# Two 64-row matmuls on the two halves of the TensorE array, in a kernel of causal convolution and rational feed-forward

## The chip, the cores and the metric

One NeuronCore of a Trainium2 chip runs the kernel. The metric is the device time of one execution in microseconds (us), the median of three runs. Durations of single instructions come from one execution that was recorded by the hardware profiler.

## What is computed

For every token and each of 8 heads, softmax weights over 7 taps mix the token's own 24 values of the head with those of the six tokens before it (zeros ahead of a sequence). The result, 16,384 rows of 192 values, goes through a feed-forward stage whose activation is a ratio of polynomials.

```python
w = exp(weight_gen - max); w = w / (sum(w) + 1e-9)          # (4, 4096, 8, 7)
out[b, s, h, :] = sum_k w[b, s, h, k] * x_pad[b, s + k, h, :]  # x (4, 4096, 192), 6 zeros ahead
h = out.reshape(16384, 192) @ w_in                            # w_in (192, 2048)
P = a[0] + a[1] * h + a[2] * h**2 + a[3] * h**3
Q = 1.0 + abs(b[0]) * abs(h) + abs(b[1]) * h**2
g = P / (Q + 1e-06)
return g @ w_out                                              # w_out (2048, 192)
```

## The kernel before, in words

**Tiles.** Each of the 128 partitions holds 128 tokens; a tile takes 4 tokens of each, 512 in all (`COLS`), so there are 32 tiles. The 2048 hidden units are 16 chunks of 128, in six groups of 3, 2, 3, 3, 2 and 3 chunks (`GROUP_CHUNKS`). A chunk's h is 128 units x 512 tokens, one PSUM bank; six banks (`hps`) hold two groups in turn, two more (`ops`) the output of the tile.

**The first product.** The 192 inputs are split in 128 and 64. To keep precision, weights and inputs are each split into a part that the fast float32r format holds exactly (hi) and a rest (lo). The 64-row remainder of the inputs stands in one tensor, `xt_hl`: hi in partitions 0 to 63, lo in 64 to 127, and the 64 last rows of the weights (`wi_hi[:, 1]`, `wi_lo[:, 1]`) are there twice, once in each half. Each chunk so takes five matmuls of 128 rows (`first_product`, L669 to L681): hi·hi, lo·hi and hi·lo of the first 128 inputs, then `wi_hi[:, 1]` and, as the fifth, `wi_lo[:, 1]` against `xt_hl`. The fifth so adds lo·hi from the upper half and lo·lo, the smallest term, from the lower. A matmul instruction loads its own weights first (LDWEIGHTS, "PEld" in the rows).

**The order of work.** It is written out by hand for each engine, with semaphores between them. In `tile` (L696) TensorE does for each group q: the transposes of the next tile's inputs, where they are due (`transpose1` at q = 1, `transpose0` at q = 4), the first product of group q, and the second product of the group four places earlier (`back`, L725, `second_product`, L683: per chunk four matmuls with 192 columns, L690). Before group q it waits until VectorE has used the h of group q-2 (`h_used`, L705). Before the second product at q = 4 it waits until ScalarE has copied the previous tile's output out of `ops` (`out_ready`, L729). That copy (`evacuate`, L441) stands in ScalarE's order at q = 3, after the Ln of L452, and waits for TensorE's second product at q = 3.

**The other engines.** ScalarE (ACT) reads a group's h three times where the square goes through it (q = 0, 2, 3, 5: L471, L474, L479) and twice otherwise (L476, L479), and inverts the denominator two groups back (`invert`, L449: L452 and L455). It waits for the h at the first of these (`h_ready`) and for the gate of the group four back (`gate_ready`, L466). VectorE (DVE) finishes the gate of the group three back (L605), does two steps of the numerator (L621, L624), and, for q = 1 and 4, a product of the denominator (L629). `lo_part1` (L570) writes the lo half of `xt_hl` for the next tile, at q = 1, ahead of that group's gate. GpSimd (POOL) does the convolution (L323, L327), the other step of the denominator (L353) and issues the accumulating DMAs (L346).

Of the kernel before, what the change touches and what calls it, by code (L numbers as in the profile page):

```python
# [25 lines left out]
F32R = mybir.dt.float32r  # L26
# [4 lines left out]
P = 128  # L31
GROUP_CHUNKS = (3, 2, 3, 3, 2, 3)
GROUPS = len(GROUP_CHUNKS)
GROUP_START = tuple(sum(GROUP_CHUNKS[:q]) for q in range(GROUPS))
# [14 lines left out]
def conv_rational_ffn(nc, x, weight_gen, w_in, w_out, a, b, out):  # L49
# [7 lines left out]
    COLS = TOK * P  # L57
    HALO = TAPS - 1
    D1 = D - P
# [19 lines left out]
    with ctx:  # L79
        def sb(name, shape, dt=F32):  # L80
            return ctx.enter_context(nc.sbuf_tensor(name, shape, dt))

        def sem(name):
            return ctx.enter_context(nc.semaphore(name))


        wi_hi = sb("wi_hi", [P, 2, FF], F32R)
        wi_lo = sb("wi_lo", [P, 2, FF], F32R)
# [14 lines left out]
        xt_hi = [sb(f"xt_hi{n}", [P, COLS], F32R) for n in range(2)]  # L103
        xt_lo = [sb(f"xt_lo{n}", [P, COLS], F32R) for n in range(2)]
        xt_hl = [sb(f"xt_hl{n}", [P, COLS], F32R) for n in range(2)]
        num = sb("num", [P, RING, GW])

        wi_stage = num[:, :, :].rearrange("p r w -> p (r w)")[:, 0:2 * FF].rearrange("p (n f) -> p n f", n=2)
# [7 lines left out]
        hps = ctx.enter_context(nc.psum_tensor("hps", [P, 6, COLS], F32))  # L116
# [6 lines left out]
        def place(odd, q, lag=0):  # L123

            return (GROUPS * odd + q - lag) % (2 * GROUPS)
# [50 lines left out]
        xt_ps1 = sem("xt_ps1")  # L176
        xt_hi_ready = sem("xt_hi_ready")
        xt_lo_ready = sem("xt_lo_ready")
        h_ready = sem("h_ready")
        abs_ready = sem("abs_ready")  # L180
        lin_ready = sem("lin_ready")
# [324 lines left out]
        def _(dve):  # L506
# [5 lines left out]
            def pre_softmax_start(s, parity):  # L512

                dve.wait_ge(taps_loaded[parity], after_dmas(s, parity))
                dve.tensor_reduce(out=tap_max[parity][:, :], in_=per_head(taps_raw[parity]), op=ALU.max,
                                  axis=AX.X).then_inc(pre_max, 1)
                dve.wait_ge(pre_max, s + 1)
                dve.tensor_tensor(per_head(taps[parity]), per_head(taps_raw[parity]), over_taps(tap_max[parity]),
                                  ALU.subtract).then_inc(pre_sub, 1)
# [50 lines left out]
            def lo_part1(s, parity, bank):  # L570

                dve.wait_ge(xt_hi_ready, 2 * s + 1)
                dve.tensor_tensor(xt_hl[parity][D1:P, :], bank[0:D1, :],
                                  xt_hl[parity][0:D1, :].bitcast(F32), ALU.subtract).then_inc(xt_lo_ready, 1)

            pre_softmax_start(0, 0)
            pre_softmax_start(1, 1)
# [12 lines left out]
            dve.wait_ge(conv_steps, CONV_STEPS)  # L590
            pre_softmax_start(2, 0)
            lo_part1(0, 0, hps[:, BANK1, :])
            lo_part0(0, 0)
            wi_lo_half(1)
# [13 lines left out]
            def tile(t, odd, first=False, xt_ahead=True, taps_ahead=True):  # L608
                for q in range(GROUPS):
# [4 lines left out]
                    if first and q == FIRST_XT1 - 1:  # L614
                        lo_part1(t + 1, 1 - odd, ops[:, 0, :])
                    if xt_ahead and q == XT1 and not first:
                        lo_part1(t + 1, 1 - odd, hps[:, BANK1, :])
# [35 lines left out]
        @block.tensor  # L653
        def _(pe):
            def transpose0(parity):

                for j in range(TOK):
                    last = pe.transpose(hps[:, BANK0, j * P:(j + 1) * P],
                                        conv[parity][:, j * D:j * D + P], ident[:, :])
                last.then_inc(xt_ps0, 1)  # L660

            def transpose1(parity, bank):

                for j in range(TOK):
                    last = pe.transpose(bank[0:D1, j * P:(j + 1) * P],  # L665
                                        conv[parity][:, j * D + P:(j + 1) * D], ident[:, :])
                last.then_inc(xt_ps1, 1)

            def first_product(q, parity, very_first=False):  # L669

                for n in range(GROUP_CHUNKS[q]):
                    units = slice((GROUP_START[q] + n) * P, (GROUP_START[q] + n + 1) * P)
                    to = hps[:, 3 * (q % 2) + n, :]
                    terms = ((wi_hi[:, 0, units], xt_hi[parity]), (wi_lo[:, 0, units], xt_hi[parity]),
                             (wi_hi[:, 0, units], xt_lo[parity]), (wi_hi[:, 1, units], xt_hl[parity]),
                             (wi_lo[:, 1, units], xt_hl[parity]))
                    for m, (w, xt) in enumerate(terms):
                        if very_first and n == 0 and m == 2:
                            pe.wait_ge(xt_lo_ready, 2)
                        last = pe.matmul(to, w, xt[:, :], start=(m == 0), stop=(m == len(terms) - 1))  # L680
                last.then_inc(h_ready, 1)  # L681

            def second_product(g):  # L683


                q = g % GROUPS
                for n in range(GROUP_CHUNKS[q]):
                    c = GROUP_START[q] + n
                    for j in range(TOK):
                        last = pe.matmul(ops[:, j // 2, (j % 2) * D:(j % 2 + 1) * D],  # L690
                                         gate[:, g % GATE_RING, n * COLS + j * P:n * COLS + (j + 1) * P],
                                         wo[:, c, :], start=(c == 0 and j % 2 == 0), stop=(c == CHUNKS - 1),
                                         skip_group_check=True)
                last.then_inc(gate_used, 1)

            def tile(t, odd, first=False, xt_ahead=True):  # L696
                if first:
                    pe.wait_ge(wi_lo_ready, 1)
                    pe.wait_ge(xt_hi_ready, 2)
                else:  # L700
                    pe.wait_ge(xt_lo_ready, 2 * t + 2)
                for q in range(GROUPS):
                    i = GROUPS * t + q
                    if not first or q >= 2:
                        pe.wait_ge(h_used, i - 1)  # L705
                    if first and GROUP_START[q] == CHUNKS // 2:
                        pe.wait_ge(wi_lo_ready, 2)
                    if xt_ahead and q == (FIRST_XT1 if first else XT1):
                        pe.wait_ge(conv_steps, CONV_STEPS * (t + 2))
                        if first:  # L710
                            pe.wait_ge(conv_by_dve, 2 * CONV_STEPS)
                        pe.sem_inc(pe_passed, 1)
                        transpose1(1 - odd, ops[:, 0, :] if first else hps[:, BANK1, :])
                    if xt_ahead and not first and q == XT1 + 2:
                        pe.wait_ge(xt_lo_ready, 2 * t + 3)
                    if xt_ahead and q == XT0:
                        transpose0(1 - odd)
                    first_product(q, odd, first and q == 0)
                    if first and q == LAG:
                        pe.wait_ge(xt_lo_ready, 3)  # L720
                        pe.wait_ge(wo_loaded, 16)
                    if not first or q >= LAG:
                        back(t, odd, q, first)

            def back(t, odd, q, first=False):  # L725

                pe.wait_ge(gate_ready, GROUPS * t + q - LAG + 1)
                if q == LAG and not first:
                    pe.wait_ge(out_ready, t)  # L729
                second_product(place(odd, q, LAG))  # L730

            pe.wait_ge(ident_ready, 2)
            pe.wait_ge(conv_steps, CONV_STEPS)
            pe.wait_ge(conv_by_dve, CONV_STEPS)
            transpose1(0, hps[:, BANK1, :])
            transpose0(0)
            tile(0, 0, first=True)
            with pe.Fori(1, TILES - 1, 2) as t:
                tile(t, 1)
                tile(t + 1, 0)  # L740
            tile(TILES - 1, (TILES - 1) % 2, xt_ahead=False)
            for q in range(LAG):
                back(TILES, TILES % 2, q)
# [21 lines left out]
```

## Time and profile before

| | |
|---|---|
| median of 3 runs | 1422.62 us (1420.06 to 1422.7) |
| the profiled execution | 1420.86 us |
| its span, first to last instruction | 1419.1 us |
| PE (TensorE matmul) | 1307.0 us busy, 92% |
| PEld (weight loads) | 1178.2 us, 83% |
| ACT | 1270.7 us, 90% |
| DVE | 1214.8 us, 86% |
| POOL | 1036.6 us, 73% |
| mean granted TensorE clock | 0.992 |

The busy times are those of the whole span. Matmuls are pipelined: the recorded duration of one is longer than the distance to the next, so a rate is read from the starts. The page's chain (the work that ended last, followed back) gives 62% of the span to PE, 25% to ACT, 7% to "issue" (time in which the engine waited for nothing that the profile shows) and 4% to DVE.

### The profile page before, as it was taken

What the parts mean: (1) busy time and instruction counts of PE and PEld (TensorE: products, weight loads), DVE (VectorE), ACT (ScalarE), POOL (GpSimd) and SP (SyncE); (2) the same over time, 40 slices, a digit from 0 to 9 for tenths busy, and PEclk for the clock granted to TensorE, in tenths of its full rate; (3) what the DMA queues carried; (4) which work ended last, traced back from release to release, by engine and by line L of the source; (5) the groups of instructions that cost most, each with busy time, mean ns of one, the idle gap of its engine ahead of it and who ended that gap; (6) DMA issues with size and microseconds to landing.
All of it is one profiled execution on the core that took longest, in us unless ns stands there. A gap on an engine that the chain in (4) does not pass through costs nothing.

```text
span 1419.1 us, 19150 instructions
## 1 busy us (share of the span) xinstructions
PE 1307.0 (92%) x6912; PEld 1178.2 (83%) x6912; DVE 1214.8 (86%) x872; ACT 1270.7 (90%) x1030; POOL 1036.6 (73%) x672
## 2 busy tenths in 40 slices
PE   0279999999999999999999999999999999999997
PEld 0268898888898888889888888988888888888897
DVE  2988898899889889989888998988988898898775
ACT  1278999999999999999999999999999999999995
POOL 1878787787878778878777887877788787787210
PEclk9889999999999999999999999999999999999999
DMA  2534444534544544454454354445345445533432
GB/s 89 144 90 110 103 117 114 128 85 107 131 94 114 125 117 88 115 120 105 109 131 107 87 126 108 117 109 131 87 102 131 97 117 120 119 83 81 100 68 67
DMA packets 35486, 152.21 MB, mean 107 GB/s; under 512 B 3992, under 2 KB 10260, under 8 KB 35472
## 3 DMA queue, kind: packets, MB, share of 16 engines
q0 software_dynamic: 18432, 100.67, 34.9%
q1 hardware_dynamic: 16752, 51.36, 10.5%
q8 instruction: 7, 0.11, 0.0%
q10 hardware_dynamic: 288, 0.00, 0.0%
q14 instruction: 7, 0.06, 0.0%
HBM read 38.78 MB, written 12.58 MB: 36 GB/s over the span
## 4 chain that ended last, share of the span: by engine, by line
PE 62%; ACT 25%; issue 7%; DVE 4%; DMA 2%; SPq 0%; ACTq 0%; DVEq 0%
PE ops L690 33%; PE hps L680 28%; ACT num L479 7%; ACT beta L474 6%; ACT den L452 6%; ACT den L471 4%; DMA xwin<-in_x 2%; ACT out_sb L446 2%; PE hps L665 1%; DVE gate L543 1%; DVE conv L554 1%; ACT den L455 1%; DVE gate L605 0%; DVE wi_lo L561 0%; DVE num L621 0%
## 5 line engine op out<-in xcount | busy, mean ns | idle before, releaser
L690 PE MATMUL ops<-wo,gate 128*128 128x192 f32 x4096 | 702.2, 327 | 41.7 <-ACT out_sb L446 35.8
L690 PEld LDWEIGHTS ops<-wo,gate 128*128 128x128 f32 x4096 | 676.0, 191 | 69.8 <-issue 48.5
L621 DVE TENSOR_TENSOR num<-num,hps 128x1536 f32<-128x1536 f32 (+1 forms) x192 | 301.6, 1571 | 153.4 <-ACT num L479 153.4
L327 POOL TENSOR_TENSOR conv<-conv,prod 128x768 f32<-128x768 f32 (+2 forms) x192 | 395.2, 2058 | 15.0
L605 DVE SCALAR_TENSOR_TENSOR gate<-num,coef,den 128x1536 f32<-128x1536 f32 (+1 forms) x192 | 375.0, 1953 | 2.6 <-issue 1.6
L323 POOL TENSOR_TENSOR prod<-xwin,taps 128x768 f32<-128x768 f32 (+2 forms) x192 | 336.7, 1754 | 3.4
L624 DVE SCALAR_TENSOR_TENSOR num<-num,coef,hps 128x1536 f32<-128x1536 f32 (+1 forms) x192 | 314.2, 1637 | 6.8
L346 POOL DMA_DIRECT2D den<-beta x128 | 112.7, 881 | 265.8 <-ACT beta L474 260.3
L479 ACT ACTIVATE num<-hps,coef 128x1536 f32<-128x1536 f32 (+1 forms) x192 | 287.8, 1499 | 0.0
L452 ACT ACTIVATE den<-den,one_eps 128x1536 f32<-128x1536 f32 (+1 forms) x192 | 277.8, 1447 | 0.0
L471 ACT ACTIVATE den<-hps,absb 128x1536 f32<-128x1536 f32 x128 | 196.6, 1536 | 77.1 <-PE hps L680 70.5
L455 ACT ACTIVATE den<-den 128x1536 f32<-128x1536 f32 (+1 forms) x192 | 259.0, 1349 | 4.2
L680 PE MATMUL hps<-xt_hi,wi_hi 128*128 128x512 f32 x512 | 226.0, 441 | 2.8 <-ACT xt_hi L415 2.8
L680 PE MATMUL hps<-xt_lo,wi_hi 128*128 128x512 f32 x512 | 203.1, 397 | 0.0
L680 PE MATMUL hps<-xt_hi,wi_lo 128*128 128x512 f32 x512 | 203.0, 397 | 0.0
L680 PE MATMUL hps<-xt_hl,wi_lo 128*128 128x512 f32 x512 | 203.0, 396 | 0.0
L680 PE MATMUL hps<-xt_hl,wi_hi 128*128 128x512 f32 x512 | 202.7, 396 | 0.0
L474 ACT ACTIVATE beta<-hps,root 128x1536 f32<-128x1536 f32 x128 | 196.8, 1538 | 0.0
L353 POOL TENSOR_SCALAR beta<-den,absb 128x1024 f32<-128x1024 f32 x64 | 136.6, 2134 | 41.3 <-ACT den L476 24.8
L680 PEld LDWEIGHTS hps<-xt_lo,wi_hi 128*128 128x128 f32 x512 | 96.9, 189 | 23.3 <-DVE xt_lo L567 0.5
L680 PEld LDWEIGHTS hps<-xt_hl,wi_hi 128*128 128x128 f32 x512 | 97.1, 190 | 22.7
L680 PEld LDWEIGHTS hps<-xt_hl,wi_lo 128*128 128x128 f32 x512 | 97.0, 189 | 22.8
(52 smaller groups left out, 766.5 us busy)
## 6 DMA issues: line engine op xcount, KB each, us to landing
den<-beta POOLq DMA_DIRECT2D x128, 768.0 KB, 5.6
xwin<-in_x SPq DMA_DIRECT2D x30, 960.0 KB
out<-out_sb SPq DMA_DIRECT2D x32, 384.0 KB, 3.8
taps_raw<-in_weight_gen SPq DMA_DIRECT2D x32, 112.0 KB, 3.9
wo<-in_moe_w_out SPq DMA_DIRECT2D x1, 1536.0 KB, 13.6
num<-in_moe_w_in SPq DMA_DIRECT2D x2, 512.0 KB, 6.6
num<-in_moe_w_in SPq DMA_DIRECT2D x4, 256.0 KB, 7.9
xwin<-in_x SPq DMA_DIRECT2D x1, 768.0 KB
```

Source lines behind the costliest of these rows:

```text
L323: pool.tensor_tensor(to[:, first_head:, :], shifted(xwin[parity], k)[:, first_head:, :], tap(taps[parity], k)[:, first_head:, :], ALU.mult ...
L327: pool.tensor_tensor(conv[parity][:, cols], conv[parity][:, cols], prod[k % 2][:, cols], ALU.add).then_inc(conv_steps, 1)
L452: act.activation(slot(den, g), slot(den, g), ACT.Ln, bias=one_eps[:, 0:1]).then_inc(ln_ready, 1)
L455: act.activation(slot(den, g), slot(den, g), ACT.Exp, scale=-1.0).then_inc(inv_q_ready, 1)
L471: act.activation(slot(den, g), h_of(q), ACT.Abs, scale=absb[:, 0:1]).then_inc(abs_ready, 1)
L474: act.activation(slot(beta, g), h_of(q), ACT.Square, scale=root[:, 2:3]).then_inc(square_ready, 1)
L479: act.activation(slot(num, g), h_of(q), ACT.Identity, scale=coef[:, 3:4], bias=coef[:, 2:3]).then_inc(lin_ready, 1)
L605: dve.scalar_tensor_tensor(slot(gate, g), slot(num, g), coef[:, 0:1], slot(den, g), ALU.add, ALU.mult).then_inc(gate_ready, 1)
L621: dve.tensor_tensor(slot(num, g), slot(num, g), h_of(q), ALU.mult).then_inc(num2_ready, 1)
L624: dve.scalar_tensor_tensor(slot(num, g), slot(num, g), coef[:, 1:2], h_of(q), ALU.add, ALU.mult).then_inc(h_used, 1)
L680: last = pe.matmul(to, w, xt[:, :], start=(m == 0), stop=(m == len(terms) - 1))
L690: last = pe.matmul(ops[:, j // 2, (j % 2) * D:(j % 2 + 1) * D], gate[:, g % GATE_RING, n * COLS + j * P:n * COLS + (j + 1) * P], wo[:, c, ...
```

## The change

The fifth matmul of the first two chunks of every group takes 64 rows in place of 128. Chunk 0's uses partitions 0 to 63 (`wi_lo` times the hi half of `xt_hl`); chunk 1's uses partitions 64 to 127, against a new tensor `xt_h2`, whose lower half holds a copy of the same hi half. The two follow each other directly and write two banks. The third chunk of a group keeps its fifth matmul of 128 rows. For the copies VectorE gets one more instruction a tile, behind the one in `lo_part1`. For chunks 0 and 1 the term lo·lo is no longer added.

```diff
@@ VectorE, lo_part1
                 dve.tensor_tensor(xt_hl[parity][D1:P, :], bank[0:D1, :],
                                   xt_hl[parity][0:D1, :].bitcast(F32), ALU.subtract).then_inc(xt_lo_ready, 1)
+                dve.tensor_copy(xt_h2[parity][D1:P, :], xt_hl[parity][0:D1, :]).then_inc(xt_h2_ready, 1)
@@ TensorE, first_product
-                for n in range(GROUP_CHUNKS[q]):
-                    units = slice((GROUP_START[q] + n) * P, (GROUP_START[q] + n + 1) * P)
-                    to = hps[:, 3 * (q % 2) + n, :]
-                    terms = ((wi_hi[:, 0, units], xt_hi[parity]), (wi_lo[:, 0, units], xt_hi[parity]),
-                             (wi_hi[:, 0, units], xt_lo[parity]), (wi_hi[:, 1, units], xt_hl[parity]),
-                             (wi_lo[:, 1, units], xt_hl[parity]))
-                    for m, (w, xt) in enumerate(terms):
-                        if very_first and n == 0 and m == 2:
-                            pe.wait_ge(xt_lo_ready, 2)
-                        last = pe.matmul(to, w, xt[:, :], start=(m == 0), stop=(m == len(terms) - 1))
+                def term(n, m, w, xt, stop=False):
+                    if very_first and n == 0 and m == 2:
+                        pe.wait_ge(xt_lo_ready, 2)
+                    return pe.matmul(hps[:, 3 * (q % 2) + n, :], w, xt, start=(m == 0), stop=stop)
+
+                def units(n):
+                    return slice((GROUP_START[q] + n) * P, (GROUP_START[q] + n + 1) * P)
+
+                def full_terms(n):
+                    term(n, 0, wi_hi[:, 0, units(n)], xt_hi[parity][:, :])
+                    term(n, 1, wi_lo[:, 0, units(n)], xt_hi[parity][:, :])
+                    term(n, 2, wi_hi[:, 0, units(n)], xt_lo[parity][:, :])
+                    term(n, 3, wi_hi[:, 1, units(n)], xt_hl[parity][:, :])
+
+                full_terms(0)
+                full_terms(1)
+                term(0, 4, wi_lo[0:D1, 1, units(0)], xt_hl[parity][0:D1, :], stop=True)
+                last = term(1, 4, wi_lo[D1:P, 1, units(1)], xt_h2[parity][D1:P, :], stop=True)
+                if GROUP_CHUNKS[q] == 3:
+                    full_terms(2)
+                    last = term(2, 4, wi_lo[:, 1, units(2)], xt_hl[parity][:, :], stop=True)
                 last.then_inc(h_ready, 1)
@@ TensorE, tile
                 if first:
                     pe.wait_ge(wi_lo_ready, 1)
                     pe.wait_ge(xt_hi_ready, 2)
+                    pe.wait_ge(xt_h2_ready, 1)
                 else:
                     pe.wait_ge(xt_lo_ready, 2 * t + 2)
+                    pe.wait_ge(xt_h2_ready, t + 1)
```

On TensorE, the first product of a group of three chunks, before (shapes are those of the outputs, 128 units x 512 tokens; `wi_hi` and `wi_lo` the weights, `xt_hi`, `xt_lo`, `xt_hl` the inputs of the tile, its parity number behind them):

```order
L680 MATMUL hps<-xt_hi1,wi_hi 128x512
L680 MATMUL hps<-xt_hi1,wi_lo 128x512
L680 MATMUL hps<-xt_lo1,wi_hi 128x512
L680 MATMUL hps<-xt_hl1,wi_hi 128x512
L680 MATMUL hps<-xt_hl1,wi_lo 128x512
L680 MATMUL hps<-xt_hi1,wi_hi 128x512
L680 MATMUL hps<-xt_hi1,wi_lo 128x512
L680 MATMUL hps<-xt_lo1,wi_hi 128x512
L680 MATMUL hps<-xt_hl1,wi_hi 128x512
L680 MATMUL hps<-xt_hl1,wi_lo 128x512
L680 MATMUL hps<-xt_hi1,wi_hi 128x512
```

and the same place now:

```order
L677 MATMUL hps<-xt_hi1,wi_hi 128x512
L677 MATMUL hps<-xt_hi1,wi_lo 128x512
L677 MATMUL hps<-xt_lo1,wi_hi 128x512
L677 MATMUL hps<-xt_hl1,wi_hi 128x512
L677 MATMUL hps<-xt_hi1,wi_hi 128x512
L677 MATMUL hps<-xt_hi1,wi_lo 128x512
L677 MATMUL hps<-xt_lo1,wi_hi 128x512
L677 MATMUL hps<-xt_hl1,wi_hi 128x512
L677 MATMUL hps<-xt_hl1,wi_lo 128x512
L677 MATMUL hps<-xt_h21,wi_lo 128x512
L677 MATMUL hps<-xt_hi1,wi_hi 128x512
```

The number of matmuls is the same; chunk 0's fifth moved behind chunk 1's fourth, next to chunk 1's fifth, and these two have 64 rows each.

On VectorE, tile 1 onward, between group q = 0's last step and group q = 1's first, before:

```order
L624 SCALAR_TENSOR_TENSOR num<-num,coef,hps 128x1536
L631 ISA
L632 TENSOR_REDUCE tap_max<-taps_raw 128x32
L572 ISA
L573 TENSOR_TENSOR xt_hl<-hps,xt_hl 64x512
L601 REGISTER_ALU
L604 REGISTER_ALU
L605 SCALAR_TENSOR_TENSOR gate<-num,coef,den 128x1024
```

and now:

```order
L627 SCALAR_TENSOR_TENSOR num<-num,coef,hps 128x1536
L634 ISA
L635 TENSOR_REDUCE tap_max<-taps_raw 128x32
L574 ISA
L575 TENSOR_TENSOR xt_hl<-hps,xt_hl 64x512
L577 COPY xt_h<-xt_hl 64x512
L604 REGISTER_ALU
L607 REGISTER_ALU
L608 SCALAR_TENSOR_TENSOR gate<-num,coef,den 128x1024
```

The copy (L577) is the one new instruction there, ahead of the gate of q = 1. Ahead of the first tile it stands between `lo_part1` and `lo_part0` in the same way.

## Rows read from the trace of the kernel before

**Rows 1.** Waits of the whole span: us in total, times, longest.
```profile
DVE num L621 <- ACT num L479: 153.4, 97, 4.0
ACT den L471 <- PE hps L680: 70.5, 64, 3.8
...
PE ops L690 <- ACT out_sb L446: 35.8, 31, 1.5
```
**Rows 2.** One tile: us; busy PE, PEld, DVE, ACT, POOL; granted clock; DMA.
```profile
677.63:719.32 41.69, 40.78 (x217) 36.52 (x217) 37.66 (x27) 39.50 (x33) 33.16 (x22) 1.00 0.47 112
```
**Rows 3.** Chain that ended last, in that tile: start us, us, what.
```profile
677.63 4.14 PE ops L690 x24
681.77 3.49 PE hps L680 x15
...
701.92 3.51 PE hps L680 x15
...
719.32 4.14 PE ops L690 x24
```
**Rows 4.** The same chain, the same step in the first and the last such tile.
```profile
135.77 4.14 PE ops L690 x24
...
1385.74 4.14 PE ops L690 x24
```
**Rows 5.** ACT's timeline in that tile; in brackets idle before, and releaser.
```profile
682.43 1.49 ACT L455 ACTIVATE den<-den 128x1536 f32<-128x1536 f32 x1
685.30 1.54 ACT L471 ACTIVATE den<-hps,absb 128x1536 f32<-128x1536 f32 x1 [1.38 <-PE hps L680]
...
703.27 1.49 ACT L455 ACTIVATE den<-den 128x1536 f32<-128x1536 f32 x1
705.45 1.54 ACT L471 ACTIVATE den<-hps,absb 128x1536 f32<-128x1536 f32 x1 [0.68 <-PE hps L680]
...
712.95 1.54 ACT L471 ACTIVATE den<-hps,absb 128x1536 f32<-128x1536 f32 x1
```
**Rows 6.** DVE's timeline in that tile; the first row is of the tile before.
```profile
675.79 1.75 DVE L621 TENSOR_TENSOR num<-num,hps 128x1536 f32<-128x1536 f32 x1 [1.43 <-ACT num L479]
...
697.19 1.75 DVE L621 TENSOR_TENSOR num<-num,hps 128x1536 f32<-128x1536 f32 x1 [1.80 <-ACT num L479]
...
701.12 0.69 DVE L573 TENSOR_TENSOR xt_hl<-hps,xt_hl 64x512 fp32r<-64x512 f32 x1
...
708.17 3.40 DVE L605 SCALAR_TENSOR_TENSOR gate<-num,coef,den 128x1536 f32<-128x1536 f32 x1
...
717.47 1.76 DVE L621 TENSOR_TENSOR num<-num,hps 128x1536 f32<-128x1536 f32 x1 [0.65 <-ACT num L479]
```
**Rows 7.** Groups by line and shape: count, busy us, mean ns, idle before.
```profile
L509 DVE MEMSET xwin<- 128x384 f32 x1 | 0.4, 378 | 0.0
```
**Rows 8.** PE and PEld in the middle of a first product, timeline.
```profile
702.22 0.39 PE L680 MATMUL hps<-xt_lo,wi_hi 128*128 128x512 f32 x1
702.22 0.19 PEld L680 LDWEIGHTS hps<-xt_hl,wi_hi 128*128 128x128 f32 x1
702.45 0.39 PE L680 MATMUL hps<-xt_hl,wi_hi 128*128 128x512 f32 x1
```
**Rows 9.** PE, then PEld, around the transposes with a 128*64 part of the array.
```profile
691.68 3.58 PE L690 MATMUL ops<-wo,gate 128*128 128x192 f32 x21
695.09 0.60 PE L665 MATMUL hps<-ident,conv 128*64 128x128 f32 x4
695.45 0.48 PE L680 MATMUL hps<-xt_hi,wi_hi 128*128 128x512 f32 x1
...
695.42 0.19 PEld L680 LDWEIGHTS hps<-xt_hi,wi_hi 128*128 128x128 f32 x1
695.53 0.19 PEld L680 LDWEIGHTS hps<-xt_hi,wi_lo 128*128 128x128 f32 x1
```
**Rows 10.** Chain that ended last, one step before the first tile.
```profile
49.29 0.69 DVE xt_hl L573
```

More of the change, by code:

```diff
@@ L105, in conv_rational_ffn @@
         xt_hl = [sb(f"xt_hl{n}", [P, COLS], F32R) for n in range(2)]
+        xt_h2 = [sb(f"xt_h2{n}", [P, COLS], F32R) for n in range(2)]
         num = sb("num", [P, RING, GW])
@@ L178, in conv_rational_ffn @@
         xt_lo_ready = sem("xt_lo_ready")
+        xt_h2_ready = sem("xt_h2_ready")
         h_ready = sem("h_ready")
```

## The prediction

> **What bounds the kernel now.** I began with the shares of the engines: PE 92%, ACT 90%, DVE 86%. So close together they name no bound, and the waits come next. [rows 1] show DVE idle 153.4 us for ACT, ACT idle 70.5 us for TensorE (64 times, two a tile) and TensorE idle only 35.8 us, 31 times, once a tile, for ACT's copy of the output. TensorE and ACT hold each other. In one tile [rows 2] TensorE's busy time is 40.78 of 41.69 us, ACT's 39.50; the granted clock is 1.00, the 2.4 GHz level.
>
> The chain of that tile [rows 3] says how. It starts at 677.63, when the output copy lets TensorE go on, and stays on TensorE to 701.92 + 3.51 = 705.43: second products and four first products, those of q = 5, 0, 1 and 2 (two of them stand in the rows, besides the last). Then it goes over to ACT, which starts on the h of q = 2 at 705.45 [rows 5], works through to the output copy, and TensorE starts again at 719.32. So 27.8 us of the 41.69 belong to TensorE, and the rest to ACT. The same step is at 135.77 in the first such tile and at 1385.74 in the last [rows 4]: 1249.97 us, 30 periods of 41.67. What a faster TensorE is worth is read from this period.
>
> Two other ways through the tile are nearly as long. **Path B:** ACT starts on q = 5 at 685.30, after 1.38 us of waiting for TensorE, then works without a gap to 703.27 + 1.49 = 704.76 and waits 0.68 us for q = 2 [rows 5]. Only one of the four first products lies ahead of that start. **Path C:** from the same start ACT feeds DVE, which begins at 697.19 [rows 6] on the numerator of q = 0 and is busy to the end of the gate at 708.17 + 3.40 = 711.57. ACT needs that gate for q = 3, which it starts at 712.95 [rows 5]: 1.38 us of slack.
>
> **The pair.** Call s what TensorE saves per group where two 64-row matmuls take the place of two of 128 rows. Matmuls of 512 columns start 0.23 us apart (702.22, 702.45) though each is recorded with 0.39 [rows 8]; a first product of three chunks takes 3.49 us for 15 [rows 3], 0.233 us each. If the two halves run side by side, one such step goes away: s = 0.23. No trace of this kernel shows two matmuls side by side, so the bounds are wide. The upper is 0.23, since the pair must take at least the one. What could eat into it is the weight loads: the pair still needs two. A load starts with the previous matmul (702.22 both) and the next matmul starts 0.23 later [rows 8]. The tightest distance of two loads in the rows is 0.11 us (695.42 to 695.53) [rows 9], so two fit into one step of 0.23 if the load for the lower half may start ahead of the matmul of the upper one. If it may not, the second matmul starts 0.11 late: s = 0.12. By the recorded length of a load, 0.19 [rows 8], s would be 0.04. The lower bound, below nothing, is in the rivals. I take 0.23: both loads go to rows that the running matmul's successor doesn't yet use, and nothing in the trace holds a load back but its place.
>
> The Trainium skill (TensorE: Matmul & The Clock Gate, "Measured speedup vs the span model") has tiles in different row groups run together at 4 ns more per further tile, which no row here shows; s would be 0.228.
>
> **What it is worth in the period.** Path A, the present chain, holds four pairs: 41.69 - 4s. Path B holds one: 41.69 - 0.68 - s = 41.01 - s. Path C holds one, and the new copy, of c us, stands in its DVE stretch, right behind the row at 701.12 [rows 6]: 41.69 - 1.38 - s + c = 40.31 - s + c. The pairs of q = 3 and 4 lie beside ACT's part of the chain; they only lengthen the wait for the output copy, 35.8 / 31 = 1.15 us a tile [rows 1], and are worth nothing.
>
> **The copy.** c is not in the trace. The nearest row is the 64x512 subtract just ahead of it, 0.69 us, which reads PSUM too [rows 6]; a write without any source takes 0.378 us for 384 columns [rows 7], 0.50 for 512 by proportion. I take 0.65, near the subtract, since both read and write the same shape. Beside a busy POOL it may be longer: the gate at 708.17 takes 3.40 us where another step of the same shape takes 1.76 [rows 6]; by that ratio c could reach 1.3. The copy is queued ahead of the gate of q = 1 and all of DVE's work up to 717.47, where DVE has 0.65 us of waiting to take it up; in the tile before, the same wait is 1.43 [rows 6], so every other tile has 0.78 more room on path C.
>
> With s = 0.23 and c = 0.65 the three paths give 40.77, 40.78 and 40.73. The period becomes **40.78**, 0.91 less by path B, and the three are tied. ACT would be busy 39.50 of it [rows 2], nearly the next bound. Thirty periods: 27.3 us.
>
> **Start and end.** Ahead of 135.77 the chain goes through three first products of tiles 0 and 1, and through one behind 1385.74: 4 x 0.23 = 0.9 less. Ahead of the first tile the chain is on DVE, and the copy stands in it, right behind the subtract at 49.29 [rows 10]: 0.65 more. Together 0.3 less. TensorE's added waits on the copy cost nothing: the copy is done right after 701.12, and the next tile's first product is due after 719.32 and the whole of q = 4 and 5. The four matmuls of chunk 1 that now come ahead of chunk 0's fifth cost nothing either: the group is handed over by one semaphore at its end, as before.
>
> **Sum.** 1420.86 - 27.3 - 0.3 = 1393.3 for the profiled execution. That stands 1.8 below the median of the runs, so I forecast **1395.0**. Own range of this case: 1389 (path B giving way a little) to 1404 (c = 1.3 lets path C bind at 41.38 in every other tile; 15 x 0.6 = 9 more).
>
> **Rivals.**
>
> *The loads come one behind the other.* s = 0.12 gives path A 41.21, path B 40.89: 0.48 a tile, 14.4 in 30, so 1408; s = 0.04 gives 0.16 a tile and 1418. For it speaks that a load never starts ahead of the previous matmul in [rows 8]; against it, that those all use the same rows of the array.
>
> *The halves don't run side by side at all,* the change then does not do what it says: s = 0, path A stays, and the copy at the start is added: 1423. Nothing in the trace speaks against it but the sense of the array; the matmuls have always been in order.
>
> *The array must run empty where the height of its parts changes,* ahead of the pair and behind it. The price is from [rows 8]: recorded 0.39, distance 0.23, so 0.16 us by which each matmul outlasts the start of the next. Twice 0.16 less the 0.23 of the pair makes s = -0.09; path A grows by 4 x 0.09 = 0.36 a tile, 30 times: 1422.6 + 10.8 + 0.65 = 1434. It decides from 0.115 us a change on. If in addition the halves don't overlap, s = -0.32 and it is 1462. Against it speaks a change of part that the trace has: the transposes with 128*64 start at 695.09, while the last of 21 second products is recorded to 691.68 + 3.58 = 695.26, and the next full matmul starts at 695.45, while the last transpose is recorded to 695.69 [rows 9]. Neither change let the array run empty. But that part is narrower, not lower, and 64 rows are not in the trace. The Trainium skill (TensorEngine Tiling (Array Packing), "Key Properties") says that changing the tiling mode, not merely the tile, drains the engine. By that rule the sum would be the 1434 of this rival; for the width of a part the trace disagrees, for the height nothing here shows it.
>
> **Chances.** Side by side with s near 0.23: 0.60. Loads in the way, 1404 to 1418: 0.14. No overlap: 0.10. Array run empty: 0.16. A measurement of this kernel tells about 0.2% from no change, 2.8 us: below 1419.8 it is faster, above 1425.5 slower. Faster is 0.60 + 0.14 = 0.74, same 0.10, slower 0.16. The range goes from 1389 to 1425 and leaves out the drained array, 0.16, and little at the low end.
>
> **What the profile would show.** If I am right: the second matmul of each pair starts within 0.02 us of the first, the three-chunk first product takes about 3.26 us in place of 3.49, the period of the output copy is 40.8, TensorE's wait for that copy grows by about 0.46 a tile, ACT's wait of 0.68 ahead of q = 2 shrinks to nearly nothing while that ahead of q = 5 stays, and DVE's of 0.65 at 717.47 is gone. The prediction is wrong if the pair's starts are 0.1 to 0.2 apart (loads) or 0.39 after the matmul before (array empty), if the step behind the pair is longer than 0.23, or if ACT is found waiting for a gate of DVE ahead of q = 3.

## The result, and the profile after

| | before | after |
|---|---|---|
| median | 1422.22 us (4 runs) | 1440.86 us (4 runs, 1440.74 to 1441.14) |
| ratio | | 1.0137, 95% interval 1.0121 to 1.0153 |
| the profiled execution, its span | 1420.86, 1419.1 | 1441.14, 1439.3 |
| PE, PEld busy | 1307.0, 1178.2 | 1331.7, 1128.6 |
| ACT, DVE busy | 1270.7, 1214.8 | 1271.0, 1231.3 |

The change costs 18.6 us. I had forecast 27 us less. The first look goes to the pair itself, in the timelines of PE and PEld after the change (start us, duration, engine, line, operands; the part of the array stands ahead of the shape):

```profile
710.90 0.40 PE L677 MATMUL hps<-xt_hl,wi_hi 128*128 128x512 f32 x1
711.23 0.50 PE L677 MATMUL hps<-xt_hl,wi_lo 64*128 64x512 f32 x1
711.24 0.49 PE L677 MATMUL hps<-xt_h,wi_lo 64*128 64x512 f32 x1
711.66 0.50 PE L677 MATMUL hps<-xt_hi,wi_hi 128*128 128x512 f32 x1
712.00 0.39 PE L677 MATMUL hps<-xt_hi,wi_lo 128*128 128x512 f32 x1
```
```profile
710.67 0.19 PEld L677 LDWEIGHTS hps<-xt_hl,wi_hi 128*128 128x128 f32 x1
711.23 0.18 PEld L677 LDWEIGHTS hps<-xt_hl,wi_lo 64*128 64x128 f32 x1 [0.37 <-issue]
711.23 0.18 PEld L677 LDWEIGHTS hps<-xt_h,wi_lo 64*128 64x128 f32 x1
711.66 0.19 PEld L677 LDWEIGHTS hps<-xt_hi,wi_hi 128*128 128x128 f32 x1 [0.24 <-issue]
711.77 0.19 PEld L677 LDWEIGHTS hps<-xt_hi,wi_lo 128*128 128x128 f32 x1
```

The two halves do start together, and both their weight loads too. But the loads, which in [rows 8] start with the matmul before, at 710.90 here, start at 711.23: 0.33 later, which is the 0.23 that the matmul takes and 0.10 more. The next full load starts 0.43 behind the pair, and the matmul behind it cannot hide that load either. From 710.90 to 712.00, where the rhythm is back, it is 1.10 us; before, with one matmul more, it was four steps of 0.233, 0.93. So the pair costs 0.17 us where it should have given 0.23. PEld's rows show the same thing as idle time: 0.37 us ahead of the pair's loads and 0.24 ahead of the next full one, here and at the other pairs of this stretch ("issue" in the brackets means that PEld waited there for no other engine).

The chain of the same kind as [rows 3], after the change (start us, us, what):

```profile
731.86 3.65 PE hps L677 x14
...
738.12 3.65 PE hps L677 x15
...
748.40 4.10 PE ops L704 x24
752.50 3.67 PE hps L677 x14
...
770.07 4.14 PE ops L704 x24
```

A first product of three chunks takes 3.65 in place of 3.49. In a group of two chunks most of the price shows behind it, in the second product at 748.40, 4.10 in place of 3.90. The first and the last tile of the chain, in place of [rows 4]:

```profile
134.48 4.14 PE ops L704 x24
...
1404.33 4.14 PE ops L704 x24
```

That is 1269.85 us for 30 tiles, 19.9 more than before; the usual tile is 727.76 to 770.07, 42.31 us. The stretches ahead of and behind the 30 tiles make 0.3 more together (1.3 less, 1.6 more), and the span is 20.2 longer. Of the 1.6, the last 64 matmuls of the second product make 1.5 (13.6 us in place of 12.1); no pair stands among them, and the granted clock was 0.78 there on the mean, against 0.88 before (1.00 is the 2.4 GHz level). In both kernels TensorE had waited 3.51 us for VectorE's gate just ahead of them. What made the 1.3 was not looked into. Four first products on the chain at 0.16 are 0.64 a tile, 19.2 in 30; two tiles from 684.68 to 770.07, in the first of which TensorE waited for DVE's gate, take 85.39 where two usual ones take 84.62, 0.8 more. That makes 20.0, against the 19.9 measured.

### The profile page after: what moved, and what is told of

It reads as the page before. It is cut to its first block, busy times and chain, and to the rows that moved or that the text cites. A ratio compares the mean times of both kernels' runs of the same rounds, so it can differ in the third digit from the quotient of the medians.

```text
span 1439.3 us, 19212 instructions
## 1 busy us (share of the span) xinstructions
PE 1331.7 (93%) x6912; PEld 1128.6 (78%) x6912; DVE 1231.3 (86%) x904; ACT 1271.0 (88%) x1030; POOL 1023.7 (71%) x672
## 4 chain that ended last, share of the span: by engine, by line
PE 61%; ACT 26%; issue 6%; DVE 4%; DMA 2%; POOL 1%; SPq 0%; ACTq 0%; DVEq 0%; POOLq 0%
PE ops L704 32%; PE hps L677 28%; ACT num L481 7%; ACT beta L476 6%; ACT den L454 6%; ACT den L473 4%; DMA xwin<-in_x 2%; ACT out_sb L448 2%; PE hps L668 1%; DVE gate L545 1%; DVE conv L556 1%; ACT den L457 1%; POOL conv L329 0%; POOL prod L325 0%; DVE gate L608 0%
## 5 line engine op out<-in xcount | busy, mean ns | idle before, releaser
L329 POOL TENSOR_TENSOR conv<-conv,prod 128x768 f32<-128x768 f32 (+2 forms) x192 | 372.0, 1938 | 15.0
L608 DVE SCALAR_TENSOR_TENSOR gate<-num,coef,den 128x1536 f32<-128x1536 f32 (+1 forms) x192 | 351.0, 1828 | 2.6 <-issue 1.6
L325 POOL TENSOR_TENSOR prod<-xwin,taps 128x768 f32<-128x768 f32 (+2 forms) x192 | 341.6, 1779 | 3.5
L677 PE MATMUL hps<-xt_hi,wi_hi 128*128 128x512 f32 x512 | 239.6, 468 | 3.8 <-DVE xt_h L577 3.8
L677 PE MATMUL hps<-xt_hl,wi_lo 64*128 64x512 f32 (+1 forms) x320 | 146.2, 457 | 0.0
L355 POOL TENSOR_SCALAR beta<-den,absb 128x1024 f32<-128x1024 f32 x64 | 113.4, 1771 | 40.8 <-ACT den L478 24.3
L677 PEld LDWEIGHTS hps<-xt_hi,wi_hi 128*128 128x128 f32 x512 | 97.3, 190 | 44.0 <-issue 35.5
L632 DVE TENSOR_TENSOR den<-den,beta 128x1024 f32<-128x1024 f32 x64 | 120.5, 1883 | 0.0
L677 PEld LDWEIGHTS hps<-xt_hl,wi_lo 64*128 64x128 f32 (+1 forms) x320 | 59.4, 186 | 76.2 <-issue 70.9
```

Source lines behind the costliest of these rows:

```text
L325: pool.tensor_tensor(to[:, first_head:, :], shifted(xwin[parity], k)[:, first_head:, :], tap(taps[parity], k)[:, first_head:, :], ALU.mult ...
L329: pool.tensor_tensor(conv[parity][:, cols], conv[parity][:, cols], prod[k % 2][:, cols], ALU.add).then_inc(conv_steps, 1)
L608: dve.scalar_tensor_tensor(slot(gate, g), slot(num, g), coef[:, 0:1], slot(den, g), ALU.add, ALU.mult).then_inc(gate_ready, 1)
L677: return pe.matmul(hps[:, 3 * (q % 2) + n, :], w, xt, start=(m == 0), stop=stop)
```

## The experiments

Twelve more kernels were run. Each was compared with the kernel before in runs on the same chip (its median lay between 1421.5 and 1421.8).

**1. Full height, with the copy.** The change's order and copy, the fifth matmuls full:

```diff
-                term(0, 4, wi_lo[0:D1, 1, units(0)], xt_hl[parity][0:D1, :], stop=True)
-                last = term(1, 4, wi_lo[D1:P, 1, units(1)], xt_h2[parity][D1:P, :], stop=True)
+                term(0, 4, wi_lo[:, 1, units(0)], xt_hl[parity][:, :], stop=True)
+                last = term(1, 4, wi_lo[:, 1, units(1)], xt_hl[parity][:, :], stop=True)
```

> Theory (the array runs empty at each change of height; weights are then loaded in the open): the fifth matmuls have 128 rows again, only their place next to each other and VectorE's copy of the change remain, so the time is that of before, 1422 to 1424 us, and a three-chunk first product takes 3.49 us. Rival (the copy on VectorE costs the time, as path C with a long copy): it stays near 1441.

Measured: 1434.92 us, ratio 1.0091 (1.0074 to 1.0108). A miss for my theory, and not what the rival said either. The copy by itself costs 13 us. The waits of this run (us in total, times, longest):

```profile
DVE num L624 <- ACT num L481: 105.5, 71, 4.0
ACT den L473 <- PE hps L677: 77.7, 64, 4.0
PEld ops L704 <- DVE gate L608: 61.6, 30, 3.8
PE ops L704 <- DVE gate L608: 48.8, 28, 3.5
```

TensorE's wait for the output copy [rows 1] is no longer among the longest, and in its place TensorE waits for VectorE's gate. The chain of one of its tiles:

```profile
666.31 0.69 DVE xt_hl L575
667.00 0.65 DVE xt_h L577
667.68 2.12 DVE gate L608
...
672.16 2.56 DVE den L632
674.73 3.56 DVE gate L608
...
678.33 4.17 PE ops L704 x24
682.50 0.44 PE hps L661 x4
682.93 2.33 PE hps L677 x10
685.26 3.90 PE ops L704 x24
```

This is a fourth path, which the prediction doesn't have. VectorE's gate at q = 2 is used first by TensorE, in the second product at q = 3, and from there TensorE needs 6.93 us (678.33 to 685.26) to the second product at q = 4. DVE's stretch from the numerator of q = 0 to the end of that gate is 15.9 us now (662.38 to 678.28). Before, it was 13.6 in all tiles between 111 and 1253 us but one, and that one is the tile of [rows 6], with 14.38 (697.19 to 711.57). What differs there is the gate of q = 1, which took 1.43 to 1.46 in the others. The odd tile, then a usual one:

```profile
701.84 2.19 DVE L605 SCALAR_TENSOR_TENSOR gate<-num,coef,den 128x1024 f32<-128x1024 f32 x1
```
```profile
1035.34 1.43 DVE L605 SCALAR_TENSOR_TENSOR gate<-num,coef,den 128x1024 f32<-128x1024 f32 x1
```

Against the usual tile, the stretch of this run is 2.3 us longer: 0.7 for the copy, 0.7 for the gate of q = 1 behind it (2.12), 0.7 for the product of the denominator (2.56 against 1.85) and 0.2 for the gate of q = 2 (3.6 against 3.4). In the change itself, with the same copy at the same place, the stretch is only 14.1 us in the usual tile, because the gate of q = 2 took 1.80 there. So what the copy does to its neighbours depends on when they run. Why was not tested.

**2. The pair without the copy.** The copy and its two waits are taken out, and chunk 1's fifth reads `xt_hl[D1:P]`.

> The copy and the waits on it are gone; the lower half of the pair reads the lo half of the inputs in place of the hi half (a term of chunk 1 is left out and lo times lo stands in its place). Theory: the pair's price stays, 1438 to 1441 us, first product 3.65 us. Rival (copy): 1422 to 1425.

Measured: 1439.05, ratio 1.0125 (1.0108 to 1.0141), as the theory has it. So the pair alone makes 17.5 us and the copy alone 13.4, but both together 18.6. They lie on two paths through the tile, and the longer counts; the fourth and fifth experiments test that.

**3. Both fifths on the same half.**

```diff
-                last = term(1, 4, wi_lo[D1:P, 1, units(1)], xt_h2[parity][D1:P, :], stop=True)
+                last = term(1, 4, wi_lo[0:D1, 1, units(1)], xt_hl[parity][0:D1, :], stop=True)
```

> Both fifth matmuls have 64 rows on the same, upper half, one behind the other; no copy. Theory: the same two changes of height, but no overlap, so 0.23 us more a group than the change; four groups lie on the chain, 0.93 a tile, 28 in 30 tiles: 1467 to 1470 us, first product 3.88 us. Rival (the two halves of the change did not really overlap either, their equal starts are an artefact of the record): about 1440, as the change.

Measured: 1470.57, ratio 1.0348 (1.0330 to 1.0365), 0.6 above the theory's range and far from the rival's 1440. The halves of the change really overlap. The tile takes 43.24 us in this run's chain (696.99 to 740.23) and 42.32 in that of the second experiment (135.01 to 177.33), which is 0.23 a group for the four groups. In PE's timeline of this run the two take 0.66 us to the next full matmul, the pair of the change 0.43:

```profile
702.60 0.40 PE L676 MATMUL hps<-xt_hl,wi_hi 128*128 128x512 f32 x1
702.92 0.73 PE L676 MATMUL hps<-xt_hl,wi_lo 64*128 64x512 f32 x2
703.58 0.50 PE L676 MATMUL hps<-xt_hi,wi_hi 128*128 128x512 f32 x1
```

**4. Pairs in groups 3 and 4 only, with the copy.** `if q in (3, 4)` around the pair, full fifths otherwise.

> Only groups q = 3 and 4, which lie beside ScalarE's part of the chain, have the pair of 64 rows; the other four have full fifth matmuls, next to each other. Theory of the paths: 2 x 0.16 us go into TensorE's wait of 1.15 us for the output copy, so 1422 to 1425 us. Rival (TensorE's total busy time sets the period): a third of the change's 18.6 us, 1428.

Measured: 1440.60, ratio 1.0130 (1.0114 to 1.0147). Theory and rival were both wrong, since both left out the price of the copy, which this run still has. The steps of its chain behind the gate are 42.38 us apart (214.62 to 257.00), those of the first experiment 42.21 (636.12 to 678.33): 0.17 more, for the pair at q = 4, which lies between gate and second product on the fourth path. The pair at q = 3 lies ahead of TensorE's wait for the gate and adds nothing. This tile is even 0.07 longer than the change's 42.31, which has four pairs more: there VectorE's stretch is the shorter one, as said under the first experiment.

**5. The same without the copy.**

> As the run with pairs in q = 3 and 4 only, but without the copy (there chunk 1's fifth reads the lo half; the term lo of the weights times hi of the inputs is left out for it). That run with the copy stood at 42.37 us a tile, the run with the copy alone at 42.22. Theory (two paths, the longer counts: the copy lengthens the one over VectorE's gate, the pairs the one over TensorE's four groups): 1420 to 1425 us, the two pairs vanish in the wait for the output copy. Rival (pairs cost wherever they stand): 1422 plus a third of 17.5, 1428.

Measured: 1421.00 (10 runs), ratio 0.9997 (0.9988 to 1.0007). Two pairs in every tile cost nothing here. The wait for the output copy takes them up, but it falls only from 35.8 us to 32.4, 0.11 a tile and not 2 x 0.16; the eleventh experiment shows where the rest is.

**6. The pair twice.**

```diff
+                term(0, 4, wi_lo[0:D1, 1, units(0)], xt_hl[parity][0:D1, :])
+                term(1, 4, wi_lo[D1:P, 1, units(1)], xt_hl[parity][D1:P, :])
                 term(0, 4, wi_lo[0:D1, 1, units(0)], xt_hl[parity][0:D1, :], stop=True)
```

> The pair is issued twice in each group, without the copy: the fifth terms are added twice, chunk 1's with the lo half of the inputs. No further change of height. Theory (the two run side by side, and inside one height the next weights load behind the running pair): 0.23 us more a group, four on the chain, 28 us over the 1439 of the single pair: 1467. If the loads are in the open for each pair, 0.34 a group: 1480. Rival (no real overlap): 0.46 a group: 1494.

Measured: 1468.46, ratio 1.0334 (1.0317 to 1.0351). In its timeline four halves take what two halves on the same side took:

```profile
704.48 0.39 PE L676 MATMUL hps<-xt_hl,wi_hi 128*128 128x512 f32 x1
704.80 0.73 PE L676 MATMUL hps<-xt_hl,wi_lo 64*128 64x512 f32 x4
705.46 0.50 PE L676 MATMUL hps<-xt_hi,wi_hi 128*128 128x512 f32 x1
```

0.66 against 0.43: a second pair costs 0.23, one step. In the tile it is the same: 43.28 us (698.88 to 742.16), 0.96 over the single pair's, 0.24 a group. Inside one height the loads hide and two matmuls go for one, as the prediction had it. The price is all in going there and coming back.

**7. The copy at q = 5.** As the first experiment, the copy moved in VectorE's order:

```diff
+                    if xt_ahead and q == 5:
+                        copy_part1(1 - odd)
                     dve.wait_ge(lin_ready, i + 1)
```

> Full fifth matmuls and the copy, as in the first experiment (1434.9 us), but the copy stands at q = 5 in VectorE's order, ahead of a step that waits for ScalarE there, and no longer ahead of the gates of q = 1 and 2. Theory (the place of the copy in VectorE's queue costs the time): 1422 to 1425. Rival (a copy costs its length wherever it stands, or the extra wait does): 1430 to 1435.

Measured: 1475.61, ratio 1.0382 (1.0365 to 1.0400). A plain miss of theory and rival. TensorE comes to the next tile's first product before VectorE has made the copy at q = 5. DVE's timeline, then PE's:

```profile
716.64 0.42 DVE L579 CAST xt_h<-xt_hl 64x512 fp32r<-64x512 f32 x1
```
```profile
717.20 0.50 PE L682 MATMUL hps<-xt_hi,wi_hi 128*128 128x512 f32 x1 [1.33 <-DVE xt_h L579]
```

The wait stands 31 times in this run, 50.5 us in all. The wait that I had costed at nothing in the change costs nothing only because the copy stood early.

**8. The output copy earlier, no pairs.** The kernel before, with `evacuate` ahead of the Ln of q = 3:

```diff
-                            if q == EVACUATE_AT and not first:
-                                evacuate(t - 1, 1 - odd, stored_needed=not second)
...
+                        if q == EVACUATE_AT and not first:
+                            evacuate(t - 1, 1 - odd, stored_needed=not second)
                         invert(i - INVERT_LAG, t if q >= INVERT_LAG else t - 1, place(odd, q, INVERT_LAG), between)
```

> The kernel before, with one thing moved: ScalarE copies the output out ahead of the Ln at q = 3, not behind it. TensorE could then go on 1.04 us sooner on the chain over its four groups. Theory of the paths: the path over VectorE's gate at q = 2 and TensorE (711.63 plus 6.93 us of second product and first product of q = 4, 718.56 against 719.32) allows 0.76 a tile, the path over ScalarE's start on q = 5 allows 0.68: 30 x 0.68 = 20 less, 1401 to 1403 us, period 41.0. Rival (TensorE or ScalarE as a whole bounds the tile): 1420 to 1423.

Measured: 1389.25, ratio 0.9775 (0.9759 to 0.9791): faster than both kernels, and by 12 us more than forecast. I had left the path over ScalarE's start on q = 5 at 41.01, but the output copy is on it too, so by the same working it falls to 39.97. For the path over the gate I had read the one odd tile of the trace. In this run too a single tile in the middle has the gate of q = 1 at 2.2 us, and TensorE waits 0.8 us for gates there; in no other tile between 120 and 1350 us does it wait for one. One tile by engine (us, busy PE, PEld, DVE, ACT, POOL, granted clock, DMA), and the end of that kernel's chain ahead of it:

```profile
745.82:786.50 40.68, 40.55 (x217) 36.63 (x217) 36.92 (x27) 39.64 (x33) 33.03 (x22) 1.00 0.49 114
```
```profile
743.37 2.33 PE hps L680 x10
745.69 0.13 issue
745.82 4.14 PE ops L690 x24
```

TensorE is now the bound, with 0.13 us of idle time left in a tile.

**9. The copy at q = 3.** As the seventh, with `q == 3`.

> Full fifth matmuls and the copy, now at q = 3 in VectorE's order: behind the gates of q = 1 and 2 on which the path over VectorE rests, ahead of a step that waits for ScalarE, and early enough for TensorE, which missed it at q = 5 by 4.1 us (the copy there ended at 717.06, the second product ahead of it at 715.7, once a tile). Theory (only the place costs): 1420 to 1425 us. Rival (a copy on VectorE costs wherever it stands): 1430 to 1435.

Measured: 1421.78 (10 runs), ratio 0.9998 (0.9988 to 1.0008). The copy costs nothing where it stands between the gate of q = 3 and a wait for ScalarE. It is also shorter there, 0.42 us at the median against 0.74 in the change, and the gate, the product and the gate that grew in the first experiment take 1.43, 1.85 and 3.40 as before. So this run does not part the place in the queue from the lengths. It does show that the new order of the matmuls and TensorE's wait on the copy, which it has too, cost nothing. In one tile in the middle the copy took 2.39:

```profile
715.82 1.82 DVE L611 SCALAR_TENSOR_TENSOR gate<-num,coef,den 128x1536 f32<-128x1536 f32 x1
717.66 2.39 DVE L579 CAST xt_h<-xt_hl 64x512 fp32r<-64x512 f32 x1
```

**10. Each half alone.** Chunk 0's 64-row fifth follows its own four terms, chunk 1's its own; no copy.

```diff
                 full_terms(0)
+                term(0, 4, wi_lo[0:D1, 1, units(0)], xt_hl[parity][0:D1, :], stop=True)
                 full_terms(1)
-                term(0, 4, wi_lo[0:D1, 1, units(0)], xt_hl[parity][0:D1, :], stop=True)
```

> Each 64-row fifth matmul stands alone, between matmuls of 128 rows, without the copy (chunk 1's reads the lo half). In the trace of the change a height section takes 0.39 us beyond its one step: 1.10 us from the start of the last full matmul to that of the second one behind, less three steps of 0.233. Theory (a price per section): 2 x 0.40 a group on the four groups of the chain, 3.2 a tile, and 0.45 more where the 1.15 us of waiting at q = 3 and 4 is used up: 30 x 3.2 = 96 to 30 x 3.65 = 110 over 1422: 1518 to 1532. Rival (the price belongs to the switch between the two halves, or to their running together): 1420 to 1445.

Measured: 1521.88, ratio 1.0708 (1.0690 to 1.0726), inside the theory's range. Its PE timeline:

```profile
704.34 0.40 PE L676 MATMUL hps<-xt_hl,wi_hi 128*128 128x512 f32 x1
704.67 0.49 PE L676 MATMUL hps<-xt_hl,wi_lo 64*128 64x512 f32 x1
705.09 0.50 PE L676 MATMUL hps<-xt_hi,wi_hi 128*128 128x512 f32 x1
705.43 0.39 PE L676 MATMUL hps<-xt_hi,wi_lo 128*128 128x512 f32 x1
```

A lone half takes the same 0.33 and 0.42 as a pair does, and full steps would have been 0.23 each. The price belongs to the change of height, not to the two running together.

**11. Pairs at q = 3 and 4 on the version with the early output copy.**

> The pairs of q = 3 and 4 alone, without the copy, which cost nothing in the kernel before (1421.0 against 1421.6), now on the version with the early output copy (1389.3), in which TensorE is busy 40.55 of 40.68 us. Theory: TensorE has no wait left to take them up, so 2 x 0.16 a tile, 10 us: 1398 to 1401. Rival (they cost nothing wherever they stand): 1388 to 1391.

Measured: 1390.10, ratio to the kernel before 0.9774 (0.9758 to 0.9790). A miss: the 0.85 us over the eighth is within the noise of 2.8 us, so the pairs are free there too. The chain of its tile:

```profile
816.61 3.63 PE hps L676 x15
820.24 3.90 PE ops L707 x24
824.14 0.44 PE hps L660 x4
824.58 2.30 PE hps L676 x10
826.87 0.01 issue
826.89 4.14 PE ops L707 x24
```

The 0.14 of q = 3 (3.63 against 3.49) went into the 0.13 that TensorE still stood idle, now 0.01. And the second product behind q = 4 takes 4.14 in both versions. Behind a wait it takes 0.24 more than the 3.90 of the others anyway, and the price of the pair's way back doesn't come on top of that. In the fifth experiment this is the part that is missing in the wait.

**12. The whole change, copy at q = 3, early output copy.**

> The change as it was made, all six pairs, with the copy moved to q = 3 and the early output copy. Theory: all six pairs are on TensorE's path, 6 x 0.16 = 0.96 a tile over 1389.3: 1417 to 1421 us; no better than the early output copy alone. Rival (with TensorE the only bound, two halves side by side pay at last): under 1389.

Measured: 1407.89, ratio 0.9906 (0.9889 to 0.9922). It is 18.6 us over the eighth (1389.25), the same as the change over the kernel before, and not the 29 that I expected: again four pairs count and those at q = 3 and 4 don't, for the reason just given. Its tile is 41.29 (1000.98 to 1042.27 in its chain), 0.6 over the eighth's, which is four times the 0.16 of a pair. The pair doesn't pay with TensorE as the only bound either. The copy at q = 3 was not run alone on this version.

## Why the prediction was wrong

**The step that failed is the size and the sign of s.** "I take 0.23: both loads go to rows that the running matmul's successor doesn't yet use, and nothing in the trace holds a load back but its place." What holds a load back is the change of height: the pair's loads start 0.33 us behind the full load's matmul, not with it, and measured s is -0.16 a group. Going from 128 rows to 64 and back costs 0.39 to 0.40 us in all (1.10 us less three steps in the change's trace, and the lone halves of the tenth experiment), against the 0.23 that the overlap gives. I read each of the two changes as some 0.10 us in which the array runs empty and some 0.10 for a weight load that nothing hides (at the way back two loads start 0.11 apart, 711.66 and 711.77). That division is read from the starts in the record; no run separated the parts, and an empty array is not seen as such.

**The overlap itself was right.** The halves start 0.01 us apart, and the third and sixth experiments show 0.23 and 0.24 us a group for it in the time of a tile. The loads of the two halves even start together, which the prediction had not dared to assume.

**The rival that came true was undersized.** "The array must run empty where the height of its parts changes" had the chance 0.16 and the time 1434. I priced a change at 0.16, by which a recorded matmul outlasts the next one's start. I left out that no weights were loaded ahead across the change. With the 0.39 measured for both changes it gives 4 x 0.16 x 30 = 19 and 1442. My argument against it was the transposes in a 128*64 part [rows 9], which are recorded to begin before the matmul ahead of them ends. That test was too weak: the pair passes it as well (710.90 + 0.40 = 711.30, past the pair's start at 711.23) and is late all the same. A better one is in the same trace, transposes at the full 128*128:

```profile
715.63 0.60 PE L658 MATMUL hps<-ident,conv 128*128 128x128 f32 x4
715.99 0.48 PE L680 MATMUL hps<-xt_hi,wi_hi 128*128 128x512 f32 x1
```

From their first start to the next full matmul is 0.36 us, as in the 128*64 part (695.09 to 695.45). So a change of width costs nothing there that the rows show, while a change of height does. The Trainium skill (TensorEngine Tiling (Array Packing), "Key Properties") has the drain at every change of the tiling mode: for the height the tenth experiment agrees, with 0.39 us for going and coming back, and for the width of the transposes the trace disagrees. I should have given more weight to a rule for which this trace had only a half-fitting counterexample. The page gives no price, but with the 0.16 that I took from the rows it would have had the sign right.

**Path A was right.** 41.69 - 4s with s = -0.16 is 42.33; the tile is 42.31. That the pairs of q = 3 and 4 are worth nothing was right too, and the fifth experiment shows it. (The rows name one other first product of that chain besides the last, not two as the prediction says; the count of four stands.)

**Path C was mis-drawn.** The gate at q = 2 has an earlier user than ScalarE at 712.95: TensorE's own second product of q = 3. In the tile that I read, that product starts at 711.63, right behind the gate's end at 711.57, and from 711.63 + 6.93 = 718.56 to 719.32 there were 0.76 us of slack, not 1.38. The tile was also the wrong one to read. "Every other tile has 0.78 more room" took the two tiles that I saw for two kinds; in the whole trace VectorE's wait of 0.65 in place of 1.4 us stands in that tile alone. In a usual tile the gate ends at 1044.31, and 0.06 + 6.93 us on from there is 1051.30, 1.5 us ahead of TensorE's restart at 1052.82. c was 0.74 us, near the 0.65 taken, but I priced its neighbours at nothing: in the first experiment they grew by 1.6 together. In the change this path was hidden by path A in all tiles but one, in which the copy took 1.49.

Had s been +0.23, the path over the gate could have been the longest: it holds two pairs (q = 5 and 4), and the first experiment's tile of 42.22 less 2 x 0.23 is 41.76, against 41.69 before and the forecast 40.78. By this estimate the change would have gained nothing with the copy where it stood. It is a weak one: no run has a free change of height, and it takes the first experiment's 3.6 us for the gate of q = 2, which was 1.80 in the change. Why the neighbours grew was not settled. DVE's product took 1.22 to 2.6 us at the same shape in these runs, and GpSimd works beside it; no run took GpSimd away.

**The small terms.** Start and end were forecast at 0.3 less and came to 0.3 more, but that nearness is luck: the parts, 1.3 less and 1.6 more, are not the terms that I had. The waits on the copy cost nothing in the 30 tiles, as said; the only one in the trace ends at 51.03, ahead of the first tile's first product. The range ended at 1425 because I left the true rival, with its chance of 0.16, outside it.

## What to carry to other kernels

Half-height matmuls side by side do run two for one, but each trip to half height and back costs 0.4 us here. By these numbers a trip at 512 columns needs at least two pairs to gain (0.47 against 0.40), and with one it loses; that is an estimate, since no run replaced four full matmuls by two pairs.

Before adding an instruction to an engine that "has slack", find the first user of everything queued behind it, on all engines, and give it a place behind those: the same copy cost 13, 54 and 0 us at three places. And look at several tiles before taking a slack from one.

Where a chain waits on an engine for one short instruction, see what stands ahead of that instruction in the queue: moving one 0.7 us copy ahead of a 1.04 us step gained 32 us, more than the whole change was meant to.

## What was not expected of the hardware

The two halves' weight loads start in the same moment (711.23 both), and the four loads of two pairs take 0.30 us together in the sixth experiment, so in these rows a load to one half doesn't wait for one to the other. Transposes in a part of less width, 128*64, take no longer than at full width (0.36 us to the next matmul in both), while a change of height costs 0.2 each way. Behind a wait for another engine the second product takes 4.14 to 4.17 in place of 3.90 for its 24 matmuls in the tiles read, and a change of height ahead of that restart added nothing to it in the eleventh experiment.
